# A fused attention and mixing kernel: which path follows the run-time branch, and two small moves in the first microseconds

## The reference

```python
B, H, S, D = 4, 8, 768, 64
scores = q @ k.T / sqrt(D)                       # per batch and head
keep = (pos_k < n_sink) | ((rel >= 0) & (rel < window))
a = exp(where(keep, scores, -1e9) - rowmax);  a /= a.sum() + 1e-9
x = (a @ v), heads side by side                  # (4, 768, 512)
theta = x @ w_theta
y = w_tok_r @ (x * cos(theta)) + w_tok_i @ (x * sin(theta))
u = x + y;  m = u + relu(u @ w_ch)
gate = sigmoid(causal 5-tap convolution of m along the sequence)
out = (gate * (m @ w_val)) @ w_out               # all float32
```

## Time and profile before

| what | value |
|---|---|
| median of 3 runs | 658.62 us (657.51 to 659.02) |
| the profiled execution, its own time | 657.9 us |
| its span, first to last instruction | 656.3 us |
| granted TensorE clock, mean | 0.994 |
| PE busy | 642.2 us (98%) |
| PEld busy | 549.2 us (84%) |
| DVE busy | 417.7 us (64%) |
| ACT busy | 295.7 us (45%) |
| POOL busy | 251.9 us (38%) |

### The profile page before, as it was taken

One profiled execution on the slowest core, in us unless ns is written; L12 is line 12 of the kernel. 1 busy time (PEld: TensorE's weight loads), 2 busy tenths in 40 slices (PEclk: granted clock), 3 DMA queues, 4 the chain that ended last, 5 costly groups with the idle time before them and its releaser, 6 DMA issues.

```text
span 656.3 us, 14120 instructions
## 1 busy us (share of the span) xinstructions
PE 642.2 (98%) x4016; PEld 549.2 (84%) x4016; DVE 417.7 (64%) x1008; ACT 295.7 (45%) x777; POOL 251.9 (38%) x322
## 2 busy tenths in 40 slices
PE   7999999999899999999999999999999999999995
PEld 5777777777688888888888888899999999999993
DVE  4887877878765365544646357869757557458450
ACT  6877877777443232232242323443344244243231
POOL 4745655555032212231131311356445445445420
PEclk9999999999999999999999999999999999999998
DMA  7667567675321136213522246330520220120011
GB/s 241 215 210 248 193 219 242 190 241 189 114 64 34 36 93 192 64 32 96 168 56 64 80 134 205 113 113 1 192 97 33 65 96 33 64 96 32 17 48 53
DMA packets 61337, 76.71 MB, mean 117 GB/s; under 512 B 4208, under 2 KB 41328, under 8 KB 61296
## 3 DMA queue, kind: packets, MB, share of 16 engines
q1 hardware_dynamic: 61296, 76.24, 36.1%
HBM read 51.06 MB, written 25.17 MB: 116 GB/s over the span
## 4 chain that ended last, share of the span: by engine, by line
PE 95%; issue 1%; DMA 1%; DVE 1%; POOL 0%; SPq 0%; POOLq 0%; ACT 0%; DVEq 0%
PE acc L1506 31%; PE ps_p L1555 18%; PE ps_th L1495 10%; PE ps_o L1595 10%; PE ps_s L503 8%; PE ps_t L529 7%; PE ps_y L552 7%; PE ps_o L566 2%; PE ps_x L1484 2%; PE ps_o L568 1%; DMA q_sb<-qT 1%; DMA x_res<-xT_scratch 1%; POOL g_lo L1148 0%; PE ps_t L512 0%; POOLq L110 0%
## 5 line engine op out<-in xcount | busy, mean ns | idle before, releaser
L1116 POOL TENSOR_TENSOR z_lo<-z_raw,z_hi 128x512 fp32r<-128x512 f32 x47 | 61.4, 1326 | 207.8 <-ACT z_hi L1193 207.8
L1506 PE MATMUL acc<-w2h,z_hi 128*128 128x512 f32 (+1 forms) x384 | 131.2, 342 | 0.0
L1506 PE MATMUL acc<-w2l,z_hi 128*128 128x512 f32 (+1 forms) x384 | 129.3, 337 | 0.0
L1506 PE MATMUL acc<-w2h,z_lo 128*128 128x512 f32 (+1 forms) x384 | 129.3, 337 | 0.0
L333 ACT ACTIVATE probs<-masked,neg_max 128x260 f32<-128x260 f32 (+1 forms) x192 | 92.6, 484 | 34.1 <-DVE neg_max L402 34.0
L402 DVE CUSTOM_DVE_ANT_0 masked<-ps_s,mask 128x260 f32<-128x260 f32 (+1 forms) x192 | 68.8, 403 | 34.7 <-PE ps_s L503 31.6
L1506 PEld LDWEIGHTS acc<-w2h,z_lo 128*128 128x128 f32 x384 | 72.8, 190 | 8.0
L1506 PEld LDWEIGHTS acc<-w2h,z_hi 128*128 128x128 f32 x384 | 72.8, 190 | 7.9
L1506 PEld LDWEIGHTS acc<-w2l,z_hi 128*128 128x128 f32 x384 | 72.9, 190 | 7.8
L1309 DVE TENSOR_TENSOR xT_lo<-ps_x,xT_hi 128x512 fp32r<-128x512 f32 x24 | 16.6, 690 | 79.0 <-ACT xT_hi L1177 79.0
L1419 DVE SCALAR_TENSOR_TENSOR ps_g<-m_raw,conv_w,ps_g 128x384 f32<-128x384 f32 x112 | 62.0, 616 | 0.2
(11 more groups left out here) (95 smaller groups left out, 1427.2 us busy)
## 6 DMA issues: line engine op xcount, KB each, us to landing
v_sb<-vP SPq DMA_DIRECT2D x16, 384.0 KB, 4.8
x_scratch<-x_sb SPq DMA_DIRECT2D x16, 384.0 KB, 2.6
x_nat<-x_scratch SPq DMA_DIRECT2D x24, 256.0 KB, 2.8
xT_scratch<-xT_raw SPq DMA_DIRECT2D x24, 256.0 KB, 2.2
x_res<-xT_scratch SPq DMA_DIRECT2D x24, 256.0 KB, 3.2
uT_scratch<-u_sb SPq DMA_DIRECT2D x24, 256.0 KB, 2.3
uT<-uT_scratch SPq DMA_DIRECT2D x8, 768.0 KB, 4.4
out<-o_sb SPq DMA_DIRECT2D x24, 256.0 KB, 2.0
```

Of the source, the lines that this page charges most:

```text
L1116: nc.gpsimd.tensor_tensor(z_lo[s % ZR][:, part, :], z_raw[:, part, :], z_hi[s % ZR][:, part, :].bitcast(F32), ALU.subtract).then_inc(z_lo_ ...
L1506: last = nc.tensor.matmul(bank, l, r, start=first and s == 0 and m == 0 and a == 0, stop=s == T - 1 and m == 1 and a == 2, skip_group_chec ...
```

## The change

Three things are edited. The test at the branch is turned round, so that the general side lies right behind it and `fast_path` behind the general side, as the `Else`. PE's wait for the identity moves from the head of its stream in `fast_path` to its first turn. A new `Early.scalar` lets ACT wait for two columns that POOL has set and compute one exponential of a 128x1 column ahead of the branch. For that POOL gets one memset of 128x1 as its first early instruction, and a semaphore `table_ready` is added.

```diff
             def turn(n, m, sinks):
                 k = VISITS * n + m
+                if isinstance(n, int) and n == 0 and m == 0:
+                    pe.wait_ge(ident_done, 2)
                 for e in range(2):
                     pe.wait_ge(exped, SCORES * n + 4 * m + 3 + e)
...
-            pe.wait_ge(ident_done, 2)
             step(0, first=True)
...
+        self.table = place(nc, "table", [P, 2], F32, SMALL_AT + 192)
...
+    def scalar(self, act):
+        act.wait_ge(self.table_ready, 1)
+        act.activation(self.table[:, 1:2], self.table[:, 0:1], ACT.Exp)
+
     def gpsimd(self, pool, ident):
         low = -BIG * float(D) ** 0.5
         own = P + FAST_SINK
+        pool.memset(self.table[:, 0:1], 0.0).then_inc(self.table_ready, 1)
         for m in (self.mask0, self.mask1, self.mask):
...
-        with nc.If(differs == 0):
+        early.scalar(nc.scalar)
+
+        with nc.If(differs != 0):
+            attention_general(nc, early, qT, kT, vP, w2, limits, x_scr, w2h, w2l, ident, x_nat, x_in)
+            mix_alone(nc, x_scr, xT_scr, uT_scr, w2h, w2l, ident, x_nat, x_in, w3, w3h, w3l, uT0, conv, out)
+        with nc.Else():
             fast_path(nc, early, qT, kT, vP, vS, w2, x_scr, xT_scr, uT_scr, w2h, w2l, ident, x_nat, x_in, w3, w3h, w3l,
                       uT0, conv, out)
-        with nc.Else():
-            attention_general(nc, early, qT, kT, vP, w2, limits, x_scr, w2h, w2l, ident, x_nat, x_in)
-            mix_alone(nc, x_scr, xT_scr, uT_scr, w2h, w2l, ident, x_nat, x_in, w3, w3h, w3l, uT0, conv, out)
```

More of the change, by code:

```diff
@@ L1683, in __init__ @@
         self.mask = place(nc, "mask", [P, KEYS], F32, at + 512 + 1056)
-        self.q_first, self.k_first, self.q_in, self.k_in, self.v_in, self.zeroed, self.masks_step, self.masks_done, self.ident_done = (
+        self.table = place(nc, "table", [P, 2], F32, SMALL_AT + 192)
+        (self.q_first, self.k_first, self.q_in, self.k_in, self.v_in, self.zeroed, self.masks_step, self.masks_done,
+         self.ident_done, self.table_ready) = (
             ctx.enter_context(nc.semaphore(n))
             for n in ("q_first", "k_first", "q_in0", "k_in0", "v_in0", "early_zeroed", "masks_step", "masks_done",
-                      "ident_done"))
+                      "ident_done", "table_ready"))
     def sync(self, sp, qT, kT, vP):
```

## The result

The changed kernel takes 662.35 us in the median of 14 runs (659.75 to 664.61); the kernel before, run beside it, 658.58 us (14 runs). The ratio is 1.0062 (95%: 1.0045 to 1.0079), so the change costs 3.0 to 5.2 us. The forecast was 657.2 us with a range up to 659.6. The sign was missed, and the time lies outside the range.

What follows compares the result with a forecast made beforehand. PE was taken as the bound, busy 98%. Removing the exit jump (-4.29 us) and adding the start lag (+2.9), other terms 0, gave -1.4 us: 658.62 to 657.2, range 655.2 to 659.6 for 8 in 10.

Steps and rivals of the forecast that it cites:

- The exit jump: PE's jump from the fast path's end over the general side, behind the last barrier: removing it was to gain 4.29 us.
- The gap of 0.59 us at 5.75: PE's idle time before the rest of the queries at the start; a later PE start was to remove it.
- The keys of pair 1: Load asked for at 11.82 us: spare 1.7 us, less 1.0 for later issue, so PE was not to wait.
- The size of PE's jump at the start: Step pricing PE's far branch ahead of its first scores: 3.9 us taken, between 3.25 and 7.5, for a lag of 2.9.
- PE is then 3.8 - 0.6 = 3.2 us late and stays so: Step after the first scores: with a 4.19 us jump, PE's lag was to stay constant at 3.2 us.
- the fetch queues behind the inputs: Rival at PE's start branch, five input loads in flight: a 7.5 us jump gives +2.2 us, 660.8; chance 14%.
- a second cold block right behind the target: Remark within the 14% rival on fetch queueing, about code after PE's start jump: it would do the same, +2.2 us.
- the forecast's lag: PE's delay after its jump at the start, taken as 2.9 us from a 3.9 us jump.
- Short fetch: Rival: start jump 3.25 us, lag 2.3, up to 1 us saved behind the span; -2.0 to -3.3, about 656.0; chance 13%.
- the forecast's own range: Range of the main case for start jumps of 3.25 to 4.9 us: 656.3 to 658.2 us; chance 60%.

Runs made afterwards that it cites:

- the kernel with only the small moves: Kernel before plus identity wait moved to the first turn and one exponential ahead of the branch, order of paths unchanged: 658.66 us, ratio 1.0006.
- end aligned: Kernel before plus address alignment of every engine at the end of the general side, without a prefetch hint: 658.11 us, ratio 0.9991.
- early exit: Kernel before with each engine branching for itself, its far jump at the end of its own work, ahead of the last barrier: 655.0 us, ratio 0.9956.

## Why the prediction was wrong

**Right.** The identity's wait and the early exponential were put at 0, and nothing else is measured (1.0006, 0.9990 to 1.0021). The exit jump was worth 4.29 us in the profile, and 4.5 us in the times of the kernel without one. The gap of 0.59 us at 5.75 was swallowed. ACT, DVE, SP and POOL arrive before PE needs them, although they stand still too: SP's first instruction behind its branch is at 8.86 in place of 5.95. I had ACT's jump start up to 1.7 us later because of the early exponential. It doesn't: its branch stands at 2.7 (2.6 before), and the table load runs beside it until 3.52. The keys of pair 1 are not waited for. The span ends with the last barrier. What was wrong lies on the other side of the sum, in PE's start.

**The step that failed first: "The size of PE's jump at the start".** I took 3.9 us between bounds of 3.25 and 7.5; it measured 5.20. The value came from the argument that fewer engines fetch at once. What decided was the load of the input, which I had kept only as the upper bound. With no input in flight the same jump takes 3.62 us; with it, 4.97 to 5.58 us in six profiles. So the unloaded jump lies below the 3.9 that I took, and the load adds 1.3 to 2.0 us. One profile of the unloaded jump against six stands behind this, and it lies clear of all six. The load is not all that the time hangs on: behind the last barrier, with no input in flight, the jump takes 4.19 to 4.29 us.

**The step that failed next: "PE is then 3.8 - 0.6 = 3.2 us late and stays so".** I had put PE back in its old rhythm at its first instruction. But the jump brought one block of code (one q8 packet), the next was asked for only at 9.3, and PE stood again, for 2.0 us, when it came to the end of the first block in the middle of its first scores. One sentence in the rival "the fetch queues behind the inputs" named this: a second cold block right behind the target would do the same. It should have been a rival of its own, with the price of a second fetch.

**The sum again.** At the second scores the forecast's lag was 2.9 us. PE's branch began 0.4 us later (3.35, not 2.95) and took 1.3 us more (5.2, not 3.9): 4.6 us. The second standstill adds 2.0, and 6.7 were measured (12.43 less 5.75). The kernel with PE's target aligned checks this: 2.9 + 0.4 + 1.1 = 4.4 us, and 4.1 measured (9.82 less 5.75). Less the 4.3 us of the exit jump the change stands at +2.4 us there. The rival "The fetch queues behind the inputs" had said +2.2, by a single jump of 7.5 us, which didn't occur; that the numbers are close is luck in part. From there the lag grew by 1.0 us until 169 us and by 0.9 us near 475 us, to 8.6 at the barrier, which is +4.3 in the profiles, where the timed ratio gives +4.1 us. Two smaller slips stand in the prediction: with a lag of 2.3 and up to 1 us more the "Short fetch" rival ends at -3.0, not -3.3, and the forecast's own range begins at 658.62 - 2.0 = 656.6, not at 656.3. Neither changes a chance or the sign.

**Why alignment doesn't make it a gain.** Without the second standstill the jump at the start still costs 4.1 us at the second scores, and the one at the end that it replaces 4.3. Like with like it is 1.8 us slower than before. Part of this comes at once: the second scores wait 0.35 us for a bank that DVE still has to read, and the first turns are 4.8 us late (12.56 against 7.79). Its last loop branch is 6.1 us late (167.4 against 161.3); what adds to the lag in between isn't shown.

**What stays open.** PE's branch began at 3.35 and not at 2.95 because its read of the limits took 1310 ns; in four other profiles with the same order the branch stands at 2.9 to 3.0, and in two at 3.3 to 3.4, so this varies from run to run. The growth up to 169 us can't be put down to the order: the kernel with only the small moves, whose first scores are as early as before, is also 1.2 us behind the kernel before in that loop (41.9 against 40.7, 162.5 against 161.3), and its time is that of the kernel before. The 0.9 us near 475 us come with a slower load (4.32 against 3.38 us), whose reason the one test of it did not find. They aren't the order's either: profiles with the order of before have the wait for that load at 1.5 to 1.7 us (small moves alone, end aligned, early exit), and the one with the order alone turned round has it at 0.6. Neither is needed for the sign: 4.3 us saved against 6.7 us lost at the second scores makes it slower already.

The Trainium skill, "Runtime: NRT & Kernel Launch", section "Instruction fetch mechanics", says that instructions come in blocks of 256, fetched one behind the other, and that a taken branch out of the window must wait for its page. The trace agrees with both: 5204 ns for the branch, and a second standstill that is gone with the target at a multiple of 256. I had used only the half on the branch. By the half on blocks the question "how far is the target from the end of its block?" follows directly.

## What to carry to other kernels

A far taken branch has a price, 3.4 to 5.6 us on PE and 2.5 to 3.5 us on SP here, whichever way round the two sides stand. Ask of each order where the engine would stand and who works meanwhile. The best place for it is at the end of an engine's own work and ahead of the meeting of all (655.0 us); behind the meeting nothing covers it (658.0), and ahead of the first work it meets the input's load and a second cold block (662.4). If a jump must stand ahead of work, keep its target away from the end of a fetch block: that is worth 2 us here (at the block's start, and 51 instructions ahead of its end served as well). Where a row vanishes from the profile but the time stays, compare the span with the execution's own time, and before a gain is put down to an edit, ask which runs hold a fall of the clock. The mean alone doesn't tell, since an idle end at half clock lowers it too.

## What the runs showed of the hardware

- A far jump of PE took 3.62 us at the start with no input load in flight, 4.97 to 5.58 us there with the input's loads, 4.19 to 4.29 us behind the last barrier, and 3.43 us at the end of PE's own work, beside a store. At the start the packet came 2.8 us after the branch in the changed kernel, and 1.2 us without the loads.
- A prefetch hint at the head of the stream was without effect (5.01 us). The one on PE near the end brought the block 14 us early and cut the jump from 4.2 to 0.33 us; those on the other four engines brought no packet ahead of the jump.
- The branch rows of DVE, ACT, POOL and SP never show their standstill (37 to 84 ns in every kernel), though SP's next instruction comes 2.5 to 3.5 us after its far branch. It must be read from the next instruction's start or, at the end, from the time around the span (1.9 to 2.2 us in the kernel before, and 4.9 where only PE was helped).
- Moving code by less than a block went with another frequency of the clock's fall in mid-run: 11 of 14 runs of the changed kernel have the lower mean, and 1 of 12 with PE's target aligned; on one chip, 5 of 5 with the order alone and 2 of 12 with all targets aligned. A fall costs 1.7 us by the trace, and 1.7 to 2.3 us by the medians of the sorted runs.
